# GpSimd subtracts the later halves of both weights' remainders itself, in place of ScalarE's negations, adding transfers and ScalarE's roundings

## The reference

```python
w = exp(weight_gen - max(weight_gen, axis=-1))         # (4, 4096, 8 heads, 7 taps)
w = w / (sum(w, axis=-1) + 1e-09)
# causal window of 7 rows of x, every head has 24 of the 192 columns
out = np.einsum('bshk,bskhg->bshg', w, x_unf)          # (16384, 192)
h = out @ w_in                                         # w_in (192, 2048)
g = h * (1.0 / (1.0 + np.exp(-1.702 * h)))
return g @ w_out                                       # w_out (2048, 192), all float32
```

## Time and profile before

| | |
|---|---|
| median of 3 runs | 1126.63 us (1126.58 to 1126.79) |
| profiled execution, its own time | 1126.67 us |
| its span (first to last recorded instruction) | 1124.9 us |
| TensorE busy | 1111.5 us, 99% |
| VectorE busy | 802.1 us, 71% |
| ScalarE busy | 622.0 us, 55% |
| GpSimd busy | 12.8 us, 1% |

### The profile page before, as it was taken

How to read it: one execution, slowest core, us unless ns; L and a number is a source line. 1 busy time by engine, 2 the same in 40 slices (tenths; PEclk the granted TensorE clock), 3 DMA queues, 4 the chain that set the end, 5 groups by cost and what they waited for, 6 DMA issues and landing times.

```text
span 1124.9 us, 21696 instructions
## 1 busy us (share of the span) xinstructions
PE 1111.5 (99%) x9748; PEld 915.3 (81%) x9748; DVE 802.1 (71%) x710; ACT 622.0 (55%) x661; POOL 12.8 (1%) x13
## 2 busy tenths in 40 slices
PE   6999999999999999999999999999999999999998
PEld 4888888888888888888888888888888888888886
DVE  7999988687685966859668496785858768587322
ACT  7767655464645555455464554645555555454543
POOL 2100000000000000000000000000000000000000
PEclk9999999999999999999999999999999999999999
DMA  8801010101001010010100101010010100100000
GB/s 274 238 15 54 15 54 1 39 29 40 29 2 39 29 40 29 1 57 12 40 29 18 51 1 40 29 40 29 1 40 29 40 29 1 40 29 1 29 1 29
DMA packets 9980, 43.46 MB, mean 39 GB/s; under 512 B 1120, under 2 KB 2400, under 8 KB 7584
## 3 DMA queue, kind: packets, MB, share of 16 engines
q1 hardware_dynamic: 8400, 40.51, 10.9%
q0 software_dynamic: 1488, 1.57, 0.9%
HBM read 24.77 MB, written 12.58 MB: 33 GB/s over the span
## 4 chain that ended last, share of the span: by engine, by line
PE 98%; DVE 1%; DMA 0%; issue 0%; ACTq 0%; DVEq 0%; SPq 0%; ACT 0%
PE hid L655 47%; PE acc_main L671 31%; PE acc_rest L671 21%; DMA gate<-in_x_first 0%; DVE hid L489 0%; DVE prod L483 0%; PE acc_main L622 0%; DVE hid L483 0%; DVE outs_main L511 0%; ACTq L73 0%; DVE outs_rest L552 0%; DVEq L73 0%; PE acc_rest L622 0%; SPq L199 0%; ACT outs_main L304 0%
## 5 line engine op out<-in xcount | busy, mean ns | idle before, releaser
L317 ACT ACTIVATE gate<-hid 128x1024 f32<-128x1024 f32 x256 | 263.1, 1028 | 480.0 <-PE hid L655 479.4
L568 DVE TENSOR_TENSOR gate_lo<-gate,gate_hi 128x1024 fp32r<-128x1024 f32 x256 | 312.9, 1222 | 260.6 <-ACT gate_hi L320 260.5
L655 PE MATMUL hid<-xt,w_hi 64*128 64x512 f32 x3072 | 431.5, 386 | 0.0
L655 PEld LDWEIGHTS hid<-xt,w_hi 64*128 64x128 f32 x3072 | 287.7, 184 | 61.6 <-ACT gate_hi L320 0.8
L671 PE MATMUL acc_main<-gate_hi,w 64*128 64x512 f32 x2048 | 315.8, 386 | 0.0
L320 ACT ACTIVATE gate_hi<-hid 128x1024 fp32r<-128x1024 f32 x256 | 260.7, 1018 | 0.0
L671 PEld LDWEIGHTS acc_main<-gate_hi,w 64*128 64x128 f32 x2048 | 191.9, 184 | 40.3
L655 PE MATMUL hid<-xt,w_lo 64*128 64x512 f32 x1536 | 215.8, 386 | 0.0
L671 PE MATMUL acc_rest<-gate_hi,w 64*128 64x512 f32 x1024 | 199.6, 386 | 0.0
L671 PE MATMUL acc_rest<-gate_lo,w 64*128 64x512 f32 x1024 | 199.6, 386 | 0.0
L671 PE MATMUL acc_main<-gate_lo,w 64*128 64x512 f32 x1024 | 199.6, 386 | 0.0
(11 more groups left out here) (57 smaller groups left out, 229.7 us busy)
## 6 DMA issues: line engine op xcount, KB each, us to landing
xwin<-in_x_runs SPq DMA_DIRECT2D x15, 1056.0 KB, 4.9
out<-outs_main SPq DMA_DIRECT2D x13, 512.0 KB, 2.6
out<-outs_rest SPq DMA_DIRECT2D x13, 256.0 KB, 2.9
taps<-in_tap_runs SPq DMA_DIRECT2D x1, 3136.0 KB, 10.4
taps<-in_w_rows SPq DMA_DIRECT2D x2, 1536.0 KB, 9.6
w_hi<-w_hi SPq DMA_DIRECT2D x2, 768.0 KB, 10.4
w_lo<-w_lo SPq DMA_DIRECT2D x2, 768.0 KB, 8.7
out<-outs_main SPq DMA_DIRECT2D x6, 256.0 KB, 2.0
```

The lines of the kernel that those rows point to most:

```text
L317: nc.scalar.activation(gate[:, v % 2, :, :], hid[:, v % 2, :, :], ACT.Gelu_apprx_sigmoid).then_inc(gate_ready, 1)
L568: nc.vector.tensor_tensor(gate_lo[:, v % SLOTS, :, :], gate[:, v % 2, :, :], gate_hi[:, v % SLOTS, :, :], ALU.subtract).then_inc(gate_lo_r ...
L655: last = nc.tensor.matmul(hid[:, v % 2, h, :], w[rows, k if j else slice_of(h, k), q, f], xt[rows, j % 2, part, k, :], start=(i == 0), sto ...
```

## The change

The four new GpSimd instructions on w2 and two on w1 subtract directly. ScalarE's negations, the accumulating transfers and ScalarE's roundings of the sums go, with their semaphores. The chunks are the same; VectorE's own calls and TensorE's list stay as they are.

```diff
-            act.wait_ge(w1_hi_ready, 1)
-            nc.scalar.activation(w1_lo[:, :, 0, LATE], w1_hi[:, :, 0, LATE].bitcast(F32), ACT.Copy, scale=-1.0
-                                 ).then_inc(w1_negated, 1)
...
-                    if n in (2, 4):
-                        at = slice((n + 2) * P, (n + 4) * P)
-                        act.wait_ge(w1_added, 16)
-                        nc.scalar.activation(w1_lo[:, :, 0, at], w1_raw[:, :, at], ACT.Copy).then_inc(w1_late_ready, 1)
-                    if n == NEG_AT:
-
-                        act.wait_ge(w2_hi_ready, 3)
-                        for at, to in LATE_CHUNKS:
-                            nc.scalar.activation(w2_of(at, to, slice(D, 2 * D)), w2_of(at, to, slice(0, D)).bitcast(F32),
-                                                 ACT.Copy, scale=-1.0).then_inc(w2_negated, 1)
-                    if n in ADDED_AT:
-                        done = ADDED_AT.index(n) + 1
-                        act.wait_ge(w2_added[done - 1], 32)
-                        at, until = LATE_CHUNKS[done - 1]
-                        for to, of in ((MAIN_LO, MAIN), (REST_LO, REST_HI)):
-                            nc.scalar.activation(w2_of(at, until, to), w2_of(at, until, of, w2_raw), ACT.Copy
-                                                 ).then_inc(w2_late_ready, 1)
...
-            pool.wait_ge(w1_negated, 1)
-            pool.dma_start(w1_raw[:, :, LATE], w1_lo[:, :, 0, LATE].bitcast(F32), accum_op=ALU.add).then_inc(w1_added, 16)
-            for i, (at, to) in enumerate(LATE_CHUNKS):
-                pool.wait_ge(w2_negated, i + 1)
-                for q in range(2):
-                    pool.dma_start(w2_of(at, to, slice(0, D), w2_raw)[:, q],
-                                   w2_of(at, to, slice(D, 2 * D)).bitcast(F32)[:, q], accum_op=ALU.add
-                                   ).then_inc(w2_added[i], 16)
+            pool.wait_ge(w1_hi_ready, 1)
+            for first in (CH // 4, CH // 4 + 2):
+                cols = slice(first * P, (first + 2) * P)
+                nc.gpsimd.tensor_tensor(w1_lo[:, :, 0, cols], w1_raw[:, :, cols], w1_hi[:, :, 0, cols].bitcast(F32),
+                                        ALU.subtract).then_inc(w1_late_ready, 1)
+            pool.wait_ge(w2_hi_ready, 3)
+            for first in (SOON, SOON + 2):
+                for to, of in ((MAIN_LO, MAIN), (REST_LO, REST_HI)):
+                    nc.gpsimd.tensor_tensor(w2_of(first, first + 2, to), w2_of(first, first + 2, of, w2_raw),
+                                            w2_of(first, first + 2, of).bitcast(F32), ALU.subtract
+                                            ).then_inc(w2_late_ready, 1)
```

More of the change, by code:

```diff
@@ L21 @@
 EVICT_AT = 1
-NEG_AT, ADDED_AT = 2, (5, 6)
 MAX_AT, EXP_AT = 2, 3
@@ L129, in ffn_of_dynamic_conv @@
         w1_hi_ready, w1_lo_ready = sem("w1_hi_ready"), sem("w1_lo_ready")
-        w1_negated, w1_added, w1_late_ready = sem("w1_negated"), sem("w1_added"), sem("w1_late_ready")
+        w1_late_ready = sem("w1_late_ready")
         w1_doubled = sem("w1_doubled")
@@ L133, in ffn_of_dynamic_conv @@
         w2_hi_ready, w2_lo_ready = sem("w2_hi_ready"), sem("w2_lo_ready")
-        w2_negated, w2_added, w2_late_ready = sem("w2_negated"), [sem("w2_added_soon"), sem("w2_added_late")], sem("w2_late_ready")
+        w2_late_ready = sem("w2_late_ready")
         taps_maxed, taps_shifted, taps_exped = sem("taps_maxed"), sem("taps_shifted"), sem("taps_exped")
@@ L174, in ffn_of_dynamic_conv @@
         SOON = CH // 4
-        LATE_CHUNKS = ((SOON, SOON + 2), (SOON + 2, CH // 2))
-        LATE = slice(FH // 2, FH)
         MAIN, MAIN_LO = slice(0, P), slice(2 * P, 3 * P)
@@ L214, in _ @@
             sp.wait_ge(w2_lo_ready, 4)
-            sp.wait_ge(w2_late_ready, 2 * len(LATE_CHUNKS))
+            sp.wait_ge(w2_late_ready, 4)
             load_taps(4, LAST, taps_loaded[2])
```

## The result

The changed kernel takes 1128.62 us (median of 22 runs, 1128.29 to 1129.79), the kernel before, measured beside it, 1126.72 us (22 runs). The ratio is 1.0016, 95% interval 1.001 to 1.0022: slower by 1.9 us. The interval leaves out 1, so the loss is real. The ratio lies within the 0.2% that the prediction set as its bound, and the interval's upper end just beyond it. The span of the profiled execution is 1127.1 us. That is 2.2 us more than before, but 0.4 us of it lies ahead of everything: GpSimd's first multiplication, which waits for the first load of x, starts at 6.37 instead of 5.97.

What follows compares the result with a forecast made beforehand. The prediction took TensorE's gapless row of matmuls to bound the kernel, so only holes in it or a later start cost time. It summed 1126.67 + 1.19 + 1.3 = 1129.2 us, with a range of 1126.4 to 1130.4.

Steps and rivals of the forecast that it cites:

- The bound and the two places: TensorE's gapless row bounds the kernel; VectorE's lateness reaches it at the head's cast and at unit 2's w2 remainder.
- slack of 0.05 us: Before unit 2's second product: VectorE's w2 remainder ends at 31.11, TensorE's load starts at 31.16.
- Removed and moved work at nothing: ScalarE's 6.6 us of dropped work, the dropped transfers, and the moved w_lo copies and taps load were costed at 0.
- The disputed price: What GpSimd's subtractions cost VectorE instructions reading both operands from SBUF: between nothing and waiting out the running GpSimd instruction.
- the upper end: A VectorE instruction with both operands in SBUF waits until the running GpSimd instruction is done; the prediction took this.
- The head's term, +1.19: At the head, GpSimd's w1 pieces delay VectorE's line 445, so the cast starts 1.19 us later than 15.46.
- starts at 16.10 and ends at 16.65: At the head, line 445 wants 14.46 but waits for GpSimd's second w1 piece; the cast starts when it ends.
- The second term, +1.3: Second stretch: GpSimd's w2 pieces make line 461 1.37 us late, giving TensorE a hole of 1.3 us before unit 2's second product.
- each waiting one letting the other in: Second stretch: GpSimd's w2 pieces and VectorE's lines 425 and 568 take turns; `gate_lo` runs 25.88 to 27.11.
- the forecast's own case: VectorE waits at both places, 1129.2 us, range 1128.5 to 1129.9; chance 0.43, of which 0.31 above 1128.9.
- no contention: Rival: VectorE isn't touched and every edit is off the path, 1126.6 us (1126.3 to 1126.9); chance 0.25.
- partial: Rival: one of the two places pays, or both engines are slowed by shares, 1127.4 to 1128.4 us; chance 0.16.

Runs made afterwards that it cites:

- e10_held_small: The changed kernel with GpSimd's w1 pieces held until VectorE's first w1 remainder is done and its w2 work cut in eight instructions: 1127.48 us.
- e8_small: The changed kernel with GpSimd's w2 work cut in eight instructions of one chunk each (256 and 128 columns): 1128.49 us.

## Why the prediction was right, and where its sizes were off

- **The bound and the two places.** Right: TensorE's row is gapless, and the two holes stand behind the cast and behind the w2 remainder, nowhere else. Wrong in a small part: the slack of 0.05 us wasn't slack. It is the time from the remainder's end to the load, which stays 0.05 to 0.06 us where the load waits.
- **Removed and moved work at nothing.** Nothing in the runs speaks against it. The waits for `gate_hi` kept their 0.8 us, the w_lo copies issued at 20.59 and the load of taps at 33.43 instead of 35.60 and 44.22 met no new wait, and with all of that work of ScalarE's gone and VectorE held least (e10_held_small) the kernel was still no faster than before.
- **The disputed price.** Taking the upper end was right, and its condition, both operands in SBUF, sorted rightly every two-operand instruction that met one of GpSimd's. The rule of the Trainium skill (page "SBUF — State Buffer", section "Who interferes with whom") is borne out in these parts: held with two SBUF inputs (1.97 us for 0.55), not held with one or none (the subtractions with one operand in PSUM at 0.68 us each, the cast at 0.69), not held by a GpSimd instruction that only writes (0.55 us beside the fills). The prediction shortened it, though: the section lets an instruction with a single SBUF input off only outside the two-port modes. Line 359, with one SBUF input, was slowed from 0.18 to 0.30 us. Whether it runs in such a mode no run here shows.
- **The head's term, +1.19, measured 0.9.** The step "starts at 16.10 and ends at 16.65" was mis-sized: GpSimd's second piece ended at 16.42 − 0.40 = 16.02, the remainder 0.41 us behind it and not 0.55, and the cast started 0.07 ahead of the remainder's recorded end. 0.08 + 0.14 + 0.07 is the 0.3 us that was missing.
- **The second term, +1.3, measured 1.0.** The step "each waiting one letting the other in" held, and GpSimd's sizes were right (1.29 us for 512 columns, 0.75 for 256, against 1.26 and 0.71), but the second line 425 was not held, as it started 0.03 us ahead of GpSimd's third piece, and `gate_lo` ended 1.08 us behind that piece instead of 1.23. Together `gate_lo` ended at 27.91 − 1.28 = 26.63 in the old times, where the prediction had 27.11, 0.48 less. Line 359, which the prediction left at its old length, gave 0.12 back: 1.37 − 0.48 + 0.12 = 1.01, and with no slack to take off that is the hole measured.
- **The direction.** The 0.2% bound lay at 1128.9, between the 1129.2 forecast and the 1128.6 measured; the two terms came out 0.6 us smaller together, and that alone put the result on the other side of it. That is partly luck. Of the chance of 0.52 for a result within the bound only 0.43 − 0.31 = 0.12 belonged to the forecast's own case; the rest stood with rivals that the runs refuted, no contention (0.25) and partial (0.14) above all. The mechanism, both places and both signs were right, and 1128.6 lies in that case's own range of 1128.5 to 1129.9; that the result fell below the bound follows from the mis-sized terms and not from the argument.

## What to carry to other kernels

Work given to an idle GpSimd isn't free: look up which VectorE instructions run beside it, count those with both operands in SBUF (and look at the lengths of the others too), and price each meeting with what is left of the GpSimd instruction. Then look whether VectorE has slack at that place (idle time before its next wait, and how long before TensorE's load its result is there). 0.48 us cost TensorE nothing where VectorE had 0.45 idle, and 1.0 us went through in full where TensorE's load came 0.05 us behind the result, which is a handover and not slack. Small GpSimd pieces took about half of the price at the w2 place (1.1 to 0.6 us of waiting), and a start moved to where VectorE reads PSUM nearly all of it at the head (0.9 to about 0.1).

## What the runs showed of the hardware that I had not expected

- A held VectorE instruction doesn't need its full length once GpSimd's piece is done: 0.41 of 0.55 us, 0.24 of 0.39, 1.08 of 1.23. Each saves about 0.15 us, the fixed part that the prediction took from line 445's two sizes. A held GpSimd piece saves as much: 1.15 of 1.29 us (the third piece, behind the second line 401), 0.60 of 0.75 (the fourth, behind `gate_lo`). That it is the fixed part that runs while the instruction waits is my reading; only the sizes agree.
- A GpSimd copy, with one operand from SBUF, holds VectorE like a subtraction (1.03 us for 0.55) and was itself stretched from 0.83 to 1.15 us.
- VectorE's small scalar addition (line 359, one operand, in SBUF) took 0.30 us instead of 0.18 in every run with GpSimd's w2 subtractions, and 0.18 in those without. It looks held like the others: in the changed kernel it ends 0.04 us behind GpSimd's piece, and in e8_small, where the pieces are cut otherwise, 0.03 us behind the end of one at 27.90. Those 0.03 us are what is left of 0.18 after the same 0.15. So "both operands in SBUF" isn't the whole condition. Two other instructions with one operand from SBUF weren't held: the reduction of line 356 took 0.37 us beside a piece, the reciprocal of line 362 in e8_small 0.35 as before. What sets line 359 apart from them no run shows.

```profile
27.22 0.37 DVE L356 TENSOR_REDUCE tap_sum<-taps 128x32 f32<-128x224 f32 x1
27.63 0.30 DVE L359 TENSOR_SCALAR tap_sum<-tap_sum 128x32 f32<-128x32 f32 x1
27.96 0.35 DVE L362 RECIPROCAL tap_inv<-tap_sum 128x32 f32<-128x32 f32 x1
```
